# Lanes and places as two-operand steps on VectorE, dealt over slots of the attention rounds; two gathers behind the last sums but one

## The reference

```python
local = np.matmul(softmax(masked(q @ k.T / sqrt(D))), v)
mem_out = (phi(q) @ M_prev) / (phi(q) @ z_prev + 1e-6)
x = g * mem_out + (1 - g) * local            # [N, 512]
logits = x @ w_gate
e_idx = np.argmax(logits, axis=1)
for e in range(E):
    mask = e_idx == e
    h = np.maximum(x[mask] @ w1[e], 0.0)
    out[mask] = gate_w[mask, None] * eom[mask, e, None] * (h @ w2[e])
```

## Time and profile before

| | |
|---|---|
| median of 3 runs | 462.83 us (462.77 to 463.34) |
| the profiled execution | 464.11 us |
| its span, first to last instruction | 462.2 us |
| PE busy | 453.9 us, 98% |
| PEld busy | 355.9 us, 77% |
| DVE busy | 303.8 us, 66% |
| ACT busy | 276.9 us, 60% |
| POOL busy | 195.3 us, 42% |
| granted TensorE clock, mean | 0.998 of full speed |

### The profile page before, as it was taken

How to read it: one execution, slowest core, us unless ns; L and a number is a source line. 1 busy time by engine, 2 the same in 40 slices (tenths; PEclk the granted TensorE clock), 3 DMA queues, 4 the chain that set the end, 5 groups by cost and what they waited for, 6 DMA issues and landing times.

```text
span 462.2 us, 11671 instructions
## 1 busy us (share of the span) xinstructions
PE 453.9 (98%) x4252; PEld 355.9 (77%) x4252; DVE 303.8 (66%) x780; ACT 276.9 (60%) x622; POOL 195.3 (42%) x192
## 2 busy tenths in 40 slices
PE   8999999999999999999999999999999999999995
PEld 6677777677777777787888888888888888888884
DVE  4889898989999997877222399222237957952220
ACT  5889988999999875344222577222237837832221
POOL 7567776769889846251222111221111312221111
PEclk9999999999999999999999999999999999999999
DMA  7234433567544723647322279410117966600000
GB/s 232 83 113 143 134 105 106 191 200 221 194 119 143 239 58 98 210 124 272 129 69 69 72 242 342 171 38 13 46 48 236 326 238 193 223 1 23 23 24 37
DMA packets 44883, 64.09 MB, mean 139 GB/s; under 512 B 7198, under 2 KB 26142, under 8 KB 44832
## 3 DMA queue, kind: packets, MB, share of 16 engines
q1 hardware_dynamic: 40672, 53.81, 35.2%
q0 software_dynamic: 4160, 9.60, 6.5%
HBM read 56.77 MB, written 10.90 MB: 146 GB/s over the span
## 4 chain that ended last, share of the span: by engine, by line
PE 97%; ACT 1%; issue 1%; DVE 0%; another core or an unknown queue 0%; POOL 0%; ACTq 0%; POOLq 0%; DVEq 0%
PE S L1469 23%; PE S L1652 19%; PE S L1653 18%; PE S L1654 18%; PE STK L1469 4%; PE TP_ps L1469 4%; PE TP_ps L1465 3%; PE TP_ps L1692 2%; PE STK L1465 2%; PE STK L1687 2%; PE S L1465 1%; ACT w_hi0b L778 0%; PE TP_ps L1675 0%; DVE probs L970 0%
## 5 line engine op out<-in xcount | busy, mean ns | idle before, releaser
L749 ACT ACTIVATE probs<-probs,neg_max 128x128 f32<-128x128 f32 (+2 forms) x144 | 82.8, 582 | 5.1 <-DVE neg_max L970 4.5
L695 POOL DMA_INDIRECT out<-x_ring,slot_tok_i x23 | 26.9, 1171 | 134.9 <-ACT x_ring L835 102.9
L1652 PE MATMUL S<-w_hi,x_hi 128*128 128x512 f32 x180 | 70.2, 390 | 0.0
L1654 PE MATMUL S<-w_hi,x_lo 128*128 128x512 f32 x180 | 70.1, 389 | 0.0
L1653 PE MATMUL S<-w_lo,x_hi 128*128 128x512 f32 x180 | 70.0, 389 | 0.0
L618 POOL DMA_INDIRECT x_ring<-x_tokens,slot_tok_i x29 | 32.0, 1105 | 85.2 <-DMA out<-x_ring,slot_tok_i 67.9
L1469 PE MATMUL S<-k_pair,q_pair 64*128 64x256 f32 (+5 forms) x384 | 64.3, 442 | 0.0
L1652 PE MATMUL S<-w_hi0b,hid_hi 128*128 128x512 f32 x152 | 61.7, 406 | 0.0
L970 DVE CUSTOM_DVE_ANT_0 probs<-S,mask 128x128 f32<-128x128 f32 (+3 forms) x128 | 55.1, 487 | 6.8 <-PE S L1469 6.3
L1653 PE MATMUL S<-w_lo0b,hid_hi 128*128 128x512 f32 x152 | 59.4, 391 | 0.0
L1654 PE MATMUL S<-w_hi0b,hid_lo 128*128 128x512 f32 x152 | 59.2, 389 | 0.0
(11 more groups left out here) (230 smaller groups left out, 875.9 us busy)
## 6 DMA issues: line engine op xcount, KB each, us to landing
w_raw<-in_moe_w SPq DMA_DIRECT2D x60, 512.0 KB, 5.3
q_pair<-in_qt SPq DMA_DIRECT2D x15, 288.0 KB, 2.9
k_pair<-in_kt SPq DMA_DIRECT2D x15, 288.0 KB, 3.4
v_nat<-in_v SPq DMA_DIRECT2D x16, 256.0 KB, 3.5
x_tokens<-x_out SPq DMA_DIRECT2D x16, 256.0 KB, 2.4
x_ring<-in_moe_w SPq DMA_DIRECT2D x2, 512.0 KB, 4.9
m_aug<-in_m_aug SPq DMA_DIRECT2D x1, 648.0 KB, 6.6
m_turned<-in_m_t SPq DMA_DIRECT2D x1, 512.0 KB, 3.6
```

The lines of the kernel that those rows point to most:

```text
L695: nc.gpsimd.indirect_dma_start(out=out[:, :], out_offset=bass.IndirectOffsetOnAxis(ap=slot_tok_i[:, t:t + 1], axis=0), in_=x_ring[:, t % X ...
L749: last = nc.scalar.activation(pr, pr, ACT.Exp, bias=neg_max[:, slot, h:h + 1], scale=-1.0, accum_out=sums[g % 2][:, at, 0:1])
L1652: T.matmul(dst, hi, part(i, k)[:, cols], start=first, stop=False)
L1654: return T.matmul(dst, lo, part(i, k)[:, cols], start=False, stop=last)
```

## The change

1. POOL's lanes go. VectorE makes all twenty, now as one TENSOR_TENSOR for several tiles (n x 128 columns, iota_f and r_lane both spread out by broadcasting) instead of a TENSOR_SCALAR for each.
2. A new routing_between(g) stands in VectorE's round between read_loc(x) and the scan of slot 3. It holds two tiles of lanes in rounds 10, 11 and 13, one in round 12, so_far(2, 3) and one tile in round 14, and place_tiles(2) in round 15. Two tiles more stand in routing_ahead(13).
3. place is cut in place_tiles and place_lanes. Its TENSOR_SCALARs become SCALAR_TENSOR_TENSORs with a constant column (per_tile, less_round) as second operand; the CAST in so_far becomes a TENSOR_TENSOR (the maximum of s_far with itself).
4. so_far(2, 3) leaves routing_behind(13), place(2) leaves routing_behind(14). In round 15 place_lanes(2) is added ahead of early_tiles, and the five lanes of sequence 2 are split two and three around the tail scan instead of three and two.
5. POOL gathers the first of the three tiles where it did, the other two behind x_out of x = 14.

```diff
-            def lanes(b):
-
-                pool.wait_ge(r_consts_dve, 1)
-                pool.wait_ge(placed, b + 1)
-                for t in range(b * TPB, (b + 1) * TPB):
-                    nc.gpsimd.tensor_scalar(r_lanes[:, t, :], iota_f[:, :], r_lane[:, t:t + 1], None, ALU.is_equal).then_inc(lanes_done, 1)
...
+                    if x == G - 2:
+                        for t in range(1, EARLY_TILES):
+                            gather(t, gather_first[t], LAST * S)
...
-                elif 0 <= g - 9 - KD < 2:
-                    lanes(g - 9 - KD)
...
-                    for t in range(EARLY_TILES):
-                        gather(t, gather_first[t], LAST * S)
+                    gather(0, gather_first[0], LAST * S)
...
-                return V.tensor_copy(r_so_far[:, n, :], s_far[:, n, :])
+                return V.tensor_tensor(r_so_far[:, n, :], s_far[:, n, :], s_far[:, n, :], ALU.max)
...
+            def place(b):
+                place_tiles(b)
+                place_lanes(b)
...
-                link(V.tensor_scalar(r_part[:, ts], r_slot[:, ts], 0.5 - P / 2, 1.0 / P, ALU.add, ALU.mult))
-                link(V.tensor_scalar(r_tile_of[:, ts, E], r_part[:, ts], ROUND, -ROUND, ALU.add, ALU.add))
-                lane = V.scalar_tensor_tensor(r_lane[:, ts], r_tile_of[:, ts, E], -float(P), r_slot[:, ts], ALU.mult, ALU.add)
-                if b < 2:
-                    lane.then_inc(placed, 1)
-                else:
-                    link(lane)
+                link(V.scalar_tensor_tensor(r_part[:, ts], r_slot[:, ts], 0.5 - P / 2, per_tile[:, 0:1].broadcast_to([P, TPB]), ALU.add, ALU.mult))
+
+            def place_lanes(b):
+                ts = tiles_of(b)
+                link(V.scalar_tensor_tensor(r_tile_of[:, ts, E], r_part[:, ts], ROUND, less_round[:, 0:1].broadcast_to([P, TPB]), ALU.add, ALU.add))
+                link(V.scalar_tensor_tensor(r_lane[:, ts], r_tile_of[:, ts, E], -float(P), r_slot[:, ts], ALU.mult, ALU.add))
...
-                for t in range(b * TPB + first, b * TPB + end):
-                    V.tensor_scalar(r_lanes[:, t, :], iota_f[:, :], r_lane[:, t:t + 1], None, ALU.is_equal).then_inc(lanes_done, 1)
+                at = slice(b * TPB + first, b * TPB + end)
+                n = end - first
+                V.tensor_tensor(r_lanes[:, at, :], iota_f[:, None, :].broadcast_to([P, n, P]),
+                                r_lane[:, at][:, :, None].broadcast_to([P, n, P]), ALU.is_equal).then_inc(lanes_done, n)
...
+            def routing_between(g):
+                if g == 10:
+                    lanes(0, 0, 2)
+                elif g == 11:
+                    lanes(0, 2, 4)
+                elif g == 12:
+                    lanes(0, 4, 5)
+                elif g == 13:
+                    lanes(1, 0, 2)
+                elif g == 14:
+                    so_far(2, 3).then_inc(hot_done, 1)
+                    lanes(1, 4, 5)
+                elif g == 15:
+                    place_tiles(2)
...
                     largest(2)
+                    lanes(1, 2, 4)
...
+                    place_lanes(2)
                     early_tiles()
-                    lanes(2, 0, 3)
+                    lanes(2, 0, 2)
...
-                    so_far(2, 3).then_inc(hot_done, 1)
...
-                    place(2)
...
-                    lanes(2, 3)
+                    lanes(2, 2, 5)
...
+                if valid(g):
+                    routing_between(g)
```

More of the change, by code:

```diff
@@ L128, in memory_attention_top1_moe @@
     void_most = sb("void_most", [P, 1])
+    per_tile = sb("per_tile", [P, 1])
+    less_round = sb("less_round", [P, 1])
     r_void = sb("r_void", [P, E], bf16)
@@ L277, in memory_attention_top1_moe @@
     scale_stored = [sem(f"scale_stored{n}") for n in range(2)]
-    placed = sem("placed")
     lanes_done = sem("lanes_done")
@@ L940, in router_consts @@
                 V.memset(void_most[D:P, :], float((EARLY_TILES - 2) * P))
+                V.memset(per_tile[:, :], 1.0 / P)
+                V.memset(less_round[:, :], -ROUND)
                 V.tensor_scalar(desc[:, :], iota_i[:, 0:E], -1.0, float(E), ALU.mult, ALU.add)
@@ L1125, in place, with place_tiles @@
             def place(b):
+                place_tiles(b)
+                place_lanes(b)
+            def place_tiles(b):
                 ts = tiles_of(b)
```

## The result

| | before | after |
|---|---|---|
| median of the runs taken together on one chip | 463.88 us (12 runs, 462.77 to 466.93) | 467.78 us (12 runs, 466.90 to 471.03) |
| ratio, 95% interval | 1 | 1.009 [1.007, 1.011] |
| the profiled execution | 464.11 us | 468.81 us |
| its span | 462.2 us | 467.1 us |
| granted TensorE clock, mean | 0.998 | 0.998 |

A forecast was written before the change was run, and what follows sets the result against it. TensorE was taken as the bound, waiting on VectorE's scan of slot 3. Terms 4.76 + 0.15 = +4.9, rounded to +4.8 us on the median 462.83, gave 467.6 us; likeliest case's range 464.6 to 469.2, slower 0.80.

The forecast's parts named there:

- What bounds the kernel: TensorE, busy 98% of the span: each us the scan of slot 3 starts later than +3.34 costs TensorE a us.
- Term 1: Rounds 10 to 15, new VectorE steps between read_loc and the scan of slot 3: held by POOL's phi_T, +4.76 us.
- Term 2: Round 15, table of the first tiles: starts later because VectorE's last lanes end later, +0.15 us beyond the stalls.
- Term 3: Work taken away or reshaped (POOL's lanes, so_far moved, two-operand forms): no gain beyond what the round 14 count includes.
- Term 4: Gathers 1 and 2 behind x_out: 0 us, upper end 0.7 us; a gain excluded, TensorE's wait being for out_T.
- What would show it: Profile after: lanes of 1.1 to 1.5 us ending with phi_T, slot 3 scan near +4.4, transposes near +5.6.
- No hold: Rival: phi_T lets VectorE in about 0.5 us after its start or never holds; 462.3 to 463.0 us, chance 0.13.
- The relief wins: Rival: two-operand steps never held, VectorE in time, rounds 13 to 15 lose their delays; 1.6 us, 461.2, chance 0.07.
- An early end of the hold: phi_T's hold ends say at +3.7: two thirds of the stalls, 465 to 466 us; counted in the forecast's own case.

The follow-up runs named there:

- experiment 3: between_first: the changed kernel with routing_between called ahead of read_loc instead of behind it; 466.12 us, ratio 1.0073 against the kernel before.
- experiment 5: The changed kernel with routing_between's steps called at the head of routing_ahead, about 5 us later in the round; 463.20 us, ratio 0.9997 against the kernel before.
- experiment 7: The kernel before with only the two-operand forms (place, so_far, VectorE's own ten lanes), every step at its old place; 462.88 us, ratio 1.0005.
- experiment 1: gathers_back: the changed kernel with its three gathers together at their old place; 467.92 us, ratio 1.0109 against the kernel before.
- experiment 2: The kernel before with two gathers moved and nothing else; 463.26 us, ratio 0.9998.
- experiment 8: The kernel before with POOL's lanes one round later, two-operand forms, and so_far(2, 3), choose(2), place(2) moved or cut; 462.79 us, ratio 0.9993.
- phi_one_input: The changed kernel with POOL's phi_T made of one input, q_exp plus a constant, instead of two; 464.78 us, ratio 1.0031 against the kernel before.

## Why the prediction was right, and where its steps were off

**What bounds the kernel** held: TensorE's work stayed at 454 us, and every us by which the scan of slot 3 came later than +3.34 was a us of the round, less some 0.05 us (round 11: +1.08 for the scan, +1.03 for the round). Experiments 3 and 5 show the other side of it: a step of 0.42 us that fits the 0.29 us of idling costs nothing, a hold of 0.70 us elsewhere costs at most 0.13.

**Term 1, the stalls.** Forecast +4.76 for rounds 10 to 15; measured:

| | 10 | 11 | 12 | 13 | 14 | 15 with its table |
|---|---|---|---|---|---|---|
| forecast | +1.04 | +1.04 | +0.90 | +0.94 | +0.23 | +0.61 + 0.15 |
| measured | +1.00 | +1.03 | +0.90 | +0.90 | +0.13 | +0.61 |

The instant of release, 0.15 us ahead of phi_T's end, was read off w_lo's rows and came out at 0.14. The Trainium skill (SBUF — State Buffer, Who interferes with whom) has the later instruction wait until the first has finished, which the prediction priced at six times 0.15 us more; the trace of after decides for the row, by 0.14 us. In round 10 the lanes took 1.03 us, not 1.5, because VectorE reached them 0.66 us after phi_T's start; the round lost as much all the same, since the scan can't start before phi_T lets go, however the wait is divided. Round 14 came out 0.10 lower. The prediction set its scan at +4.42, as behind two tiles; but r_so_far (0.57 us, let go 0.15 us ahead of phi_T's end) and the tile of lanes behind it (0.28 us) are together shorter than two tiles, and the scan came at +4.36, the transposes at +5.54.

**Term 2, the table, +0.15**, is the term that was too large: round 15 with its table cost +0.61, and its transposes alone +5.46 - 4.88 = +0.58, which leaves 0.03. The last lanes (three tiles, 0.56 us) ended 7.36 us behind the start of the scan of slot 3 (168.96 to 176.32), where 7.5 was reckoned and 7.31 was the old distance, and that scan started at +4.27, not +4.31. What the term missed is room ahead of the tail scan: in the kernel before the lanes ahead of it ended at 169.38 and it started at 169.47, while a step that follows without a wait starts some 0.08 us before the end of the one ahead, so 0.17 us of the new steps cost nothing. (Its own numbers, 0.80 less 0.61, give 0.19 and not 0.15.) TensorE's wait for the lanes only grew from 0.29 to 0.37 us.

**Term 3, nothing for what is taken away.** For POOL's lanes this held. The forms are worth 0.3 us, in round 14, in the one trace of experiment 7; the prediction had this stretch inside its count for round 14 and so didn't lose it. That held forms are held by the same POOL steps is right for w_lo and the first part of q_pos and wrong for the later part of q_pos (experiment 7).

**Term 4, the gathers, 0.** The cost was 0, as experiments 1 and 2 show. But the sentence that a gain was excluded, because TensorE's wait there was for out_T, rested on a wait of one execution: 0.7 us in the profile of before and in none of the nine others, with the gathers at either place. ScalarE's copy had idled 1.68 us there for a releaser that the profile calls remote, none of the core's engines. It was no property of the kernel. The same goes for the other sign: the 1.12 us by which the profiled execution of after began its rounds later is chance as well. That the forecast for the span, +4.8, met 4.9 is in part these two (-0.79 and +1.12) cancelling; the medians, +3.9 here and +4.45 for gathers_back, stand on either side of the 4.57 of the rounds. And that 467.6 came within 0.2 us of the measured 467.78 is luck in good part: it was +4.8 on top of 462.83, and what was measured is +3.90 on top of 463.88. The sizes to go by are the stalls, 4.76 forecast and 4.57 measured. The rounding of the sum to +4.8 had no ground either: the little delay that it names for rounds 10 and 12 isn't in the trace of before, where both have their transposes at +4.56.

**What would show it** came as written: lanes of 1.39 to 1.53 us in rounds 11 to 13 that end 0.14 to 0.28 us behind phi_T, scan of slot 3 at +4.42 and transposes at +5.6 (with one tile, in round 12, +4.28 and +5.46), rounds 10, 12 and 13 at 11.33, 11.19 and 11.33 us, the wait of round 14 gone. Two items were off: the lanes of round 10 lasted 1.03 us, for the reason above, and VectorE's busy time grew by 5.2 us, not by over 6.

**The rivals.** "No hold" fell with the 1.53 us. (Its items, added up, span 0.45 us slower to 0.8 faster, not 0.2 to 0.5; the case would still have been no change.) "The relief wins" fell with it; experiments 7 and 8 put the relief, by their traces, at 0.3 us for the forms and 0.7 for what that version keeps, half of the 1.6 us that the rival gave itself. "An early end of the hold" is what phi_one_input made true; it cost 1.3 us there, less than the two thirds of the stalls that the prediction gave this case, since a hold that ends 0.5 us after phi_T's start is mostly over when the lanes come.

## What to carry to other kernels

Before a step is put into a gap of one engine, look what the engine that contends with it for SBUF does at that very time, not what the gap measures: a gap of 0.29 us took 0.42 us of work for nothing and 1.5 us of the same work at full price, and the two places were 0.9 us apart. A helper step belongs where the next thing behind it on its engine is one that nobody waits for yet: there a hold of 0.70 us cost 0.13 us at most. And a wait that stands in one profile only, of a remote releaser above all, should carry no term of a sum in either direction.

## What the runs showed of the hardware that was not expected

**How long POOL holds depends on its inputs, not on its length.** A two-input POOL step of 1.41 us held a VectorE step to 0.14 us before its end, a one-input step of 1.66 us and the same 576 columns let a two-input one through 0.52 and 0.53 us after its start.

**A one-input POOL step holds twice, and the second time only some forms.** Behind q_pos a CAST of eight columns lasted until 0.03 us after POOL's end, a TENSOR_TENSOR of the same eight columns 0.17 us (experiment 7). In round 12 of the changed kernel a TENSOR_SCALAR of eight columns did as the CAST (first row of VectorE, last of POOL):

```profile
140.79 0.56 DVE L1089 TENSOR_SCALAR r_not_far<-turn_of 128x8 bf16<-128x8 f32 x1
...
141.41 0.76 DVE L966 CUSTOM_DVE_ANT_0 probs<-S,mask_tail 128x576 f32<-128x576 f32 x1
...
139.68 1.64 POOL L587 TENSOR_SCALAR q_pos<-q_pair 128x576 f32<-128x576 f32 x1
```

Two more TENSOR_SCALARs issued right behind it ended with it. But in between_first this same step, r_not_far, took 0.17 us beside q_pos, and the next one, r_offs, lasted 0.68 us, to q_pos's end. What differs is the time: r_not_far started 0.93 us after q_pos there and 1.11 us after it here, r_offs 1.01 us. The ten traces agree on this. Of the TENSOR_SCALARs and CASTs of VectorE from SBUF to SBUF that they list beside a one-input POOL step of some 1.65 us, all 21 that started 0.57 to 0.97 us after it took their own time, and all 46 that started 1.00 to 1.44 us after it ended with it, to within 0.05 us. Of the 44 TENSOR_TENSORs and SCALAR_TENSOR_TENSORs that started in that later stretch, 36 took their own time; the other eight stood right behind a held TENSOR_SCALAR or CAST. So in its first half us the POOL step holds the one-input and the two-input forms (no CAST stands there), then none, and from 1.00 us on the TENSOR_SCALARs and CASTs alone. The element type isn't what decides: r_offs (f32 to f32) and r_not_far (f32 to bf16) are both held, the TENSOR_TENSOR from f32 to bf16 isn't. That the form has one input isn't enough either, for reductions went through at all times and so did a COPY of 240 columns at 1.01 us. More these runs don't separate.

**The hold works both ways.** VectorE's two-input w_lo0b stretched POOL's x_out from 1.58 to 2.53 us and an addition of 160 columns from 0.52 to 1.52 us.
